# The first loads of a fused attention and expert kernel: constants in three groups, smaller gate and slot weights, and a wait moved

## What is computed

```python
state = gamma[None, :, None, None] * state + np.einsum('bhd,bhe->bhde', k[:, :, t], v[:, :, t])
y[:, :, t] = scale * np.einsum('bhd,bhde->bhe', q[:, :, t], state)
...
logits = x @ w_gate
e_idx = np.argmax(logits, axis=1)
...
eom = 1.0 / (1.0 + np.exp(-(x @ w_output_gate)))
...
h = np.maximum(x[mask] @ w1[e], 0.0)
ye = h @ w2[e]
out[mask] = gate_w[mask, None] * eom[mask, e, None] * ye
...
logits = x @ phi
...
slot_input = d.T @ x
...
return (c @ slot_out).astype(np.float32)
```

## Time and profile before

| | |
|---|---|
| median of 3 runs | 594.92 us (593.11 to 595.69) |
| the profiled execution | 595.07 us, its span 593.4 us |
| mean granted clock of TensorE | 0.947 |
| PE busy | 536.0 us, 90% of the span |
| DVE, ACT, POOL busy | 250.3, 195.2, 147.1 us |

### The profile page before, as it was taken

How to read it: one execution, slowest core, us unless ns; L and a number is a source line. 1 busy time by engine, 2 the same in 40 slices (tenths; PEclk the granted TensorE clock), 3 DMA queues, 4 the chain that set the end, 5 groups by cost and what they waited for, 6 DMA issues and landing times. The chain is left out here.

```text
span 593.4 us, 10700 instructions
## 1 busy us (share of the span) xinstructions
PE 536.0 (90%) x4349; PEld 443.9 (75%) x4349; DVE 250.3 (42%) x422; ACT 195.2 (33%) x372; POOL 147.1 (25%) x145
## 2 busy tenths in 40 slices
PE   4999999953899999999999999999999999755884
PEld 3777777732799899899899899899899899611441
DVE  2456666556224353363363363264264260211343
ACT  2223242220224354354253353353354261301132
POOL 2314141304411151151152052052050041030000
PEclk9999999995699999999999999999999999969795
DMA  8899887611218319319409305405303308879939
GB/s 318 288 345 375 310 328 283 244 53 50 72 70 275 143 53 295 142 37 308 147 21 324 144 10 196 143 4 201 143 5 143 141 5 336 293 264 380 387 148 349
DMA packets 45777, 115.35 MB, mean 194 GB/s; under 512 B 5589, under 2 KB 5998, under 8 KB 45742
## 3 DMA queue, kind: packets, MB, share of 16 engines
q1 hardware_dynamic: 36654, 99.83, 46.9%
q0 software_dynamic: 5200, 7.95, 4.9%
q10 hardware_dynamic: 3888, 7.08, 3.2%
HBM read 101.00 MB, written 13.82 MB: 194 GB/s over the span
## 5 line engine op out<-in xcount | busy, mean ns | idle before, releaser
L1238 PE MATMUL bank<-xT_hi,w_hi 128*128 128x432 f32 x256 | 97.8, 382 | 1.0 <-DVE xT_lo L918 1.0
L1238 PE MATMUL bank<-hT_hi,w_hi 128*128 128x432 f32 x256 | 94.1, 368 | 0.0
L1239 PE MATMUL bank<-xT_lo,w_hi 128*128 128x432 f32 x256 | 93.0, 363 | 0.0
L1240 PE MATMUL bank<-xT_hi,w_lo 128*128 128x432 f32 x256 | 92.6, 362 | 0.0
L1239 PE MATMUL bank<-hT_lo,w_hi 128*128 128x432 f32 x256 | 92.0, 359 | 0.0
L1240 PE MATMUL bank<-hT_hi,w_lo 128*128 128x432 f32 x256 | 91.9, 359 | 0.0
L538 POOL DMA_INDIRECT slot_logits<-lcur,logit_row_of_row x32 | 39.7, 1239 | 202.3 <-DVE lcur L932 144.1
L923 DVE SCALAR_TENSOR_TENSOR hT_lo<-bank,hT_hi 128x432 fp32r<-128x432 f32 x64 | 38.9, 607 | 113.4 <-ACT hT_hi L658 111.6
L658 ACT ACTIVATE hT_hi<-bank 128x432 fp32r<-128x432 f32 x64 | 34.0, 531 | 103.2 <-PE bank L1240 100.5
L1238 PEld LDWEIGHTS bank<-xT_hi,w_hi 128*128 128x128 f32 x256 | 48.9, 191 | 9.8 <-issue 6.3
L662 ACT ACTIVATE yT<-bank 128x432 f32<-128x432 f32 x32 | 17.0, 531 | 106.6 <-PE bank L1240 106.6
(11 more groups left out here) (176 smaller groups left out, 692.1 us busy)
## 6 DMA issues: line engine op xcount, KB each, us to landing
w_raw<-in_w SPq DMA_DIRECT2D x64, 512.0 KB, 6.5
v_units<-in_v SPq DMA_DIRECT2D x13, 2048.0 KB, 15.5
qk<-in_qk SPq DMA_DIRECT2D x24, 512.0 KB, 4.4
kv<-in_kv SPq DMA_DIRECT2D x24, 512.0 KB, 5.4
x_rows<-xrow ACTq DMA_DIRECT2D x27, 256.0 KB, 3.1
out<-orow SPq DMA_DIRECT2D x12, 512.0 KB, 4.4
v<-in_v SPq DMA_DIRECT2D x2, 2048.0 KB, 19.0
v_units<-in_v SPq DMA_DIRECT2D x2, 1024.0 KB, 15.6
```

The source lines that it names most:

```text
L1238: pe.matmul(out, wh, xh, start=first_, stop=False)
L1239: pe.matmul(out, wh, xl, start=False, stop=False)
L1240: return pe.matmul(out, wl, xh, start=False, stop=last_)
```

## The change

`const` has its columns in a new order and is loaded in three pieces with a semaphore each: 149 columns for the mask and the decay (`s_const`), 256 for the identity and the slot sum (`s_turn`), and 480 for what only the routing part reads (`s_rest`). `wg` and `phi` hold their weights once. POOL no longer fills `xrow` with zeros, and ACT no longer stores them; ACT writes one column of each tile instead, which keeps the count. The copy to `const16` is made in two pieces, the second after `s_rest`. DVE waits for `yscale` where the loop first uses it.

```diff
@@ -52,16 +52,22 @@
...
-C_ID, C_SUM, C_TRI, C_ONE, C_IOTA = 0, 128, 256, 384, 512
-C_J = C_IOTA + P
-C_16, N_16 = C_TRI, 3 * P + T
-C_P = C_J + T
-C_W8 = C_P + 1
-C_RST = C_W8 + NE
-C_KD = C_RST + NE * T
+C_IOTA = 0
+C_P = C_IOTA + P
+C_KD = C_P + 1
 C_SD = C_KD + HEADS
 C_GS = C_SD + PAIRS
-C_N = C_GS + HEADS
+N_FIRST = C_GS + HEADS
+C_ID = N_FIRST
+C_SUM = C_ID + P
+N_TURN = C_SUM + P
+C_TRI = N_TURN
+C_ONE = C_TRI + P
+C_J = C_ONE + P
+C_W8 = C_J + T
+C_RST = C_W8 + NE
+C_N = C_RST + NE * T
+N_16 = 3 * P + T
...
@@ -147,7 +153,7 @@
...
         const = put("const", [C_N])
-        phi = put("phi", [KT, P])
+        phi = put("phi", [KT, SLOTS])
         idx = put("token_of_row", [TW + XW], I32)
...
@@ -200,7 +206,7 @@
...
         const16 = put("const16", [N_16], BF16, at=r)
-        wg = put("wg", [KT, P], at=r)
+        wg = put("wg", [KT, SLOTS], at=r)
         lg = put("gate_logits", [T + 1, 16], at=r)
...
@@ -299,17 +305,18 @@
...
         ident = const[:, C_ID:C_ID + P]
-        tri_less1 = const16[:, C_TRI - C_16:C_TRI - C_16 + P]
-        ones = const16[:, C_ONE - C_16:C_ONE - C_16 + P]
+        tri_less1 = const16[:, 0:P]
+        ones = const16[:, P:2 * P]
         slotsum = const[:, C_SUM:C_SUM + P]
-        iota16 = const16[:, C_IOTA - C_16:C_IOTA - C_16 + P]
-        j16 = const16[:, C_J - C_16:C_J - C_16 + T]
+        j16 = const16[:, 2 * P:2 * P + T]
+        iota16 = const16[:, 2 * P + T:]
...
         s_const, s_mask, s_ysc, s_wg, s_phi = [sem(n) for n in ("s_const", "s_mask", "s_yscale", "s_wg", "s_phi")]
+        s_turn, s_rest = sem("s_const_turn"), sem("s_const_rest")
         s_qk = [sem(f"s_qk{i}") for i in range(NB)]
...
@@ -407,15 +414,17 @@
...
                 if isinstance(i, int) and i == 0:
-                    sp.dma_start(const[:, :], const_h).then_inc(s_const, 16)
+                    sp.dma_start(const[:, 0:N_FIRST], const_h[:, 0:N_FIRST]).then_inc(s_const, 16)
                 sp.dma_start(kv[par][:, :, :], kv_h[i]).then_inc(s_kv[par], 16)
                 if isinstance(i, int) and i == 0:
+                    sp.dma_start(wg[:, :, :], wg_h).then_inc(s_wg, 16)
+                    sp.dma_start(const[:, N_FIRST:N_TURN], const_h[:, N_FIRST:N_TURN]).then_inc(s_turn, 16)
                     sp.dma_start(yscale[:, :, :], yscale_h).then_inc(s_ysc, 16)
-                    sp.dma_start(wg[:, :, :], wg_h).then_inc(s_wg, 16)
...
             sp.dma_start(phi[:, :, :], phi_h).then_inc(s_phi, 16)
+            sp.dma_start(const[:, N_TURN:], const_h[:, N_TURN:]).then_inc(s_rest, 16)
...
@@ -492,8 +501,6 @@
...
-            for par in range(2):
-                pool.memset(xrow[par][:, :], 0.0)
             pool.memset(acc[:, :], 0.0)
...
@@ -597,10 +604,12 @@
...
             for par in range(2):
-                act.dma_start(x_d[par * P:(par + 1) * P, :], xrow[par][:, :]).then_inc(s_xst[par], 16)
+                act.activation(xrow[par][:, 0:1], stat[:, 7:8], ACT.Copy).then_inc(s_xst[par], 16)
             act.activation(stat[:, 7:8], stat[:, 7:8], ACT.Copy).then_inc(s_gev, 1)
             act.wait_ge(s_const, 16)
-            act.activation(const16[:, :], const[:, C_16:C_16 + N_16], ACT.Copy).then_inc(s_c16, 1)
+            act.activation(const16[:, 2 * P + T:], const[:, C_IOTA:C_IOTA + P], ACT.Copy)
+            act.wait_ge(s_rest, 16)
+            act.activation(const16[:, 0:2 * P + T], const[:, C_TRI:C_TRI + 2 * P + T], ACT.Copy).then_inc(s_c16, 1)
             act.activation(stat[:, 6:7], stat[:, 6:7], ACT.Copy).then_inc(s_lg, 1)
...
@@ -797,7 +806,6 @@
...
             dve.wait_ge(s_mask, 1)
-            dve.wait_ge(s_ysc, 16)
             with dve.Fori(0, BATCH) as bt:
...
@@ -820,6 +828,8 @@
...
                                     (w1_low, w2_low)[kind](0, p)
+                    if c == 0:
+                        dve.wait_ge(s_ysc, 16)
                     dve.wait_ge(s_av, i + 1)
...
@@ -1146,13 +1156,13 @@
...
-                pe.wait_ge(s_const, 16)
+                pe.wait_ge(s_turn, 16)
                 pe.wait_ge(s_wg, 16)
...
                     g_ = slice(k * SLOTS, (k + 1) * SLOTS)
-                    mm = pe.matmul(bank[4][g_, 0:P], wg[:, k, g_], xT[:, k, :], start=True, stop=True)
+                    mm = pe.matmul(bank[4][g_, 0:P], wg[:, k, :], xT[:, k, :], start=True, stop=True)
                 mm.then_inc(s_gt, 1)
...
@@ -1287,7 +1297,7 @@
...
                     g_ = slice(k * SLOTS, (k + 1) * SLOTS)
-                    mm = pe.matmul(bank[6][g_, 0:TC], phi[:, k, g_], yT[:, k, :], start=True, stop=True)
+                    mm = pe.matmul(bank[6][g_, 0:TC], phi[:, k, :], yT[:, k, :], start=True, stop=True)
                 mm.then_inc(s_c1, 1)
...
@@ -1484,10 +1494,9 @@
...
     x_order = [hd * HD + d for pair in HEAD_AT for hd in pair for d in range(HD)]
-    gates = np.concatenate([inputs["moe_w_gate"], inputs["moe_w_output_gate"]] * (P // (2 * NE)), axis=1)[x_order]
-    wg = np.ascontiguousarray(gates.reshape(KT, P, P).transpose(1, 0, 2))
-    phis = np.concatenate([inputs["moe2_phi"]] * (P // SLOTS), axis=1)
-    phi = np.ascontiguousarray(phis.reshape(KT, P, P).transpose(1, 0, 2))
+    gates = np.concatenate([inputs["moe_w_gate"], inputs["moe_w_output_gate"]] * (SLOTS // (2 * NE)), axis=1)[x_order]
+    wg = np.ascontiguousarray(gates.reshape(KT, P, SLOTS).transpose(1, 0, 2))
+    phi = np.ascontiguousarray(inputs["moe2_phi"].reshape(KT, P, SLOTS).transpose(1, 0, 2))
     const, yscale = shape_constants()
...
```

## The result

| | before | after |
|---|---|---|
| median of 10 runs | 594.72 us (593.11 to 595.76) | 597.5 us (597.1 to 599.47) |
| profiled execution, its span | 595.07 us, 593.4 us | 597.65 us, 595.6 us |
| PE busy | 536.0 us | 534.8 us |

The ratio is 1.0054, with a 95% interval of 1.004 to 1.0068: slower by 2.4 to 4.0 us. That is the border of the 0.5% that I had set as no change, and clearly not zero.

A forecast was written before the change was run, and what follows sets the result against it. PE, gapless after its first chunk, was taken to bound the kernel, so a start delay reaches the end. +0.84 us for gate_sum(0) held by ACT and +0.8 for TensorE's pace made +1.6 on 594.92: 596.5 us, range 593.3 to 599.0.

The forecast's parts named there:

- The start bounds the end: Attention's first chunk on PE: moving it by x moves the end by x, less at most 0.7 us of waiting.
- kv lands earlier: First kv load, behind smaller loads: landing at 5.4 to 7.0, k-v product at 6.5 to 8.1; alone 1.9 to 3.5 us gained.
- The wait for the last group holds ACT, and ACT holds gate_sum: ACT's second constant copy, chunk 0: gate_sum(0) at 14.7 against 13.86, +0.84 us, bounds -0.8 to +2.5.
- T: Landing time of the last const group in the load queue: 13.75 us, between 12.3 and 15.15.
- the old rates: Transfer rates before the change: 130 GB/s to 3 us, 270 from 3 to 7, 415 from 7 to 13.
- The pace of TensorE: PE behind its stop before gate_sum(0): a second slow stretch costs +1.6 us or 0; half taken, +0.8.
- fast short groups in chunk 0: Sign in the profile after: PE's short groups already fast in chunk 0 would mean a time lower than forecast.
- Parts that cost nothing: yscale's later wait, POOL's zero fills with ACT's stores, and ACT's small copies: worth nothing by themselves.
- A queue slow with short rows: Rival 1, load queue: many short-rowed transfers make it slower by over 0.5%, T = 16.0, time 598.8 us; chance 0.15.
- the estimate was 2.4 us more: Load queue, by the skill's figure: the three transfers of 64 to 75 KB add about 2.4 us, near rival 1.

The follow-up runs named there:

- late copy: The changed kernel with ACT's wait for the last const group and the copy behind it moved behind ACT's attention loop; 592.76 us, ratio 0.9965.

## Why the prediction was right, and where it was short

I forecast 596.5 us, 1.6 us or 0.27% slower, between 593.3 and 599.0. It is 597.5, and 2.8 us slower by the medians. The mechanism is the one forecast. The two sizes in the sum were too small, and a third part of the loss, outside the span, wasn't in it.

- **The start bounds the end.** Right. The 2.35 us at chunk 2 are the 2.35 us at the routing part.
- **kv lands earlier.** Right, though the k-v product at 8.21 is just past my upper bound of 8.1. The rate from 3 to 7 us stayed low (269 GB/s), so the stores and the long rows of const aren't needed for slow transfers. The late copy, with the same first loads, had 361 GB/s there, so the rate isn't fixed either, and the earlier kv rests in part on the execution.
- **The wait for the last group holds ACT, and ACT holds gate_sum.** Right, shown by the chain, by undoing it (the ratio goes from 1.0054 to 0.9965, some 5.3 us) and by adding it alone to the kernel of before.
- **T.** I took 13.75: 13.35, half way between a queue at full rate and the old rates, and 0.4 for short rows. It was 14.23; the old rates alone give 14.4, with nothing for short rows. There was no reason in the rows for a faster queue. The midpoint was 1.05 too low, and the 0.4, for a slowness that wasn't seen, hid part of it. ACT's part behind it was 0.75 us, not 0.95: entering the loop showed no extra time. Together the term was +1.12 for +0.84.
- **The pace of TensorE.** I took half of 1.6, and it was 1.23 in the trace. The picture behind it differs: I had PE slow from its first work behind the stop on. In the trace gate_sum at 14.98 was fast, and the clock fell afterwards, for 3 us of work at half the clock. I had also named fast short groups in chunk 0 as a sign of a time below my forecast; gate_sum was one (0.49 us), and the time was above it. The fall follows a stop both here and in the earlier trace rows, and none shows in the late copy, where PE doesn't stop. But the run with yscale awaited late was slow for longer with no such stop, so what the stop costs on average isn't shown. The 1.23 us are those of this trace.
- **The part outside the span.** I took the end of the span for the end of the time. Some 0.4 us more lie between the two in the changed kernel. The runs of the kernel of before without the zero rows, with the late yscale or with the wait for phi don't have it (1.59 to 1.72), and all those with the grouped loads have at least 0.2, so it comes with the grouping or the smaller weights. Its cause is open.
- **Parts that cost nothing.** yscale's wait and ACT's small copies: right, as far as runs of this kind can tell. The stores I counted only as part of the earlier kv; without the wait they are the one part whose gain is clear of zero.
- **The rivals.** A queue slow with short rows was not seen: the last group came before the 14.4 us that the old rates give. The Trainium skill, "DMA: Bandwidth & Descriptors", section Bandwidth, gives 0.95 us for a transfer of 64 KB, issued from GpSimd. By that figure the estimate was 2.4 us more; the landing at 14.23 doesn't agree with it for transfers of SP in a full queue. The forecast of chances put 0.79 on less than 0.5%; the ratio of 1.0054 lies just past that line, with an interval on both sides of it.

In sum: 1.12 for gate_sum and 1.23 for pace are 2.35 at chunk 2, of which 2.2 are left at the end of the span, and 0.4 outside it make 2.6, against 2.8 by the medians. The remaining 0.2 is within what single executions differ by.

## What to carry to other kernels

When a load is split by time of use, follow each new wait down its engine's own order: a copy that nobody needs for 100 us still holds all that stands behind it. Put the wait where the data is used, or load early what an early instruction waits for. Behind a stop of PE look at the granted clock too: here it fell behind one of 2.96 us. And before a wait is priced by one trace of the start, look at a second one: behind the same queue a landing moved by 1 us, and the length of the slow stretch by 5 us, from one execution to another.

## What was not expected of the hardware

- The granted clock can fall when a stop is over: PE stood from 12.0 to 14.98, ran its first group at the fast pace (0.49 us), and was at 0.50 from 16 to nearly 19 us.
- In the first stretch of each trace the clock column reads 1.00 while the same groups of matmuls take 1.12 us instead of 0.66; there only the durations tell the pace.
- With nine matmuls on zeros ahead of the loop PE was fast on both sides of a wait of 0.9 us: the k-v product took 0.69 instead of 1.12 us.
- The same kv tile behind the same queue was there at 8.88 in one execution, at 8.32 in another and at 7.93 in a third; in the grouped queue at 7.11 and 6.35.
- PE worked at the slow pace from 9.97 to about 14.5 in the kernel of before, and from 9.03 to about 18.8, with one gap of 0.48, where only DVE's wait for yscale had been moved.
- With the grouped loads the time exceeds the span by 0.2 to 0.4 us more (by the medians), and no execution with them (1.79 and up) is as low as one without them (1.72 at most).
